# Attention, then two gated layers, on one core: q and k split together on GpSimd, with copies from SBUF to SBUF by DMA

## The reference

```python
scores = scale * np.matmul(q, k.transpose(0, 1, 3, 2))
scores = np.where(block_i >= block_j, scores, -1000000000.0)
scores = scores - np.max(scores, axis=-1, keepdims=True)
attn = np.exp(scores)
attn = attn / (np.sum(attn, axis=-1, keepdims=True) + 1e-09)
out = np.matmul(attn, v)

h = x @ w_in                                # layer 1
x = (h * np.clip(h + 3.0, 0.0, 6.0) / 6.0) @ w_out
h = x @ w2_in                               # layer 2
x = (h * np.tanh(np.log1p(np.exp(h)))) @ w2_out
```

## Time and profile before

| | us |
|---|---|
| median of 3 runs | 982.85 (982.0 to 983.21) |
| the profiled execution, its own time | 982.5 |
| its span, first to last instruction | 980.7 |
| TensorE busy (matmuls) | 949.2, 97% |
| VectorE busy | 761.2, 78% |
| ScalarE busy | 651.0, 66% |
| GpSimd busy | 446.6, 46% |

### The profile page before, as it was taken

One profiled execution on the slowest core, in us unless ns is written; L12 is line 12 of the kernel. 1 busy time (PEld: TensorE's weight loads), 2 busy tenths in 40 slices (PEclk: granted clock), 3 DMA queues, 4 the chain that ended last, 5 costly groups with the idle time before them and its releaser, 6 DMA issues.

```text
span 980.7 us, 17734 instructions
## 1 busy us (share of the span) xinstructions
PE 949.2 (97%) x6004; PEld 844.8 (86%) x6004; DVE 761.2 (78%) x1443; ACT 651.0 (66%) x1429; POOL 446.6 (46%) x409
## 2 busy tenths in 40 slices
PE   6988999999999999999999999999999999999998
PEld 5877888899888889988888988988988898998896
DVE  6999899967777576779897876777877777777654
ACT  6998899946544454554546457777777777776663
POOL 7887899876847586967776670000000000000000
PEclk9999999999999999999999999999999999999999
DMA  7878777765788977697777455455555654565255
GB/s 175 227 202 240 193 183 201 198 181 169 234 288 295 326 235 262 213 320 252 277 272 252 172 192 200 178 195 223 194 203 196 219 200 172 176 243 193 87 193 194
DMA packets 81913, 211.48 MB, mean 216 GB/s; under 512 B 12320, under 2 KB 19104, under 8 KB 81824
## 3 DMA queue, kind: packets, MB, share of 16 engines
q1 hardware_dynamic: 81744, 210.06, 65.7%
q10 hardware_dynamic: 80, 0.29, 0.1%
HBM read 170.39 MB, written 39.92 MB: 214 GB/s over the span
## 4 chain that ended last, share of the span: by engine, by line
PE 73%; DVE 5%; ACT 1%; issue 1%; DMA 1%; POOL 0%; SPq 0%; ACTq 0%; DVEq 0%
PE psum L957 36%; PE psum L840 11%; PE psum L842 11%; PE psum L841 11%; PE psum L790 1%; DVE ebuf L1511 1%; DVE glo L1517 1%; PE psum L769 1%; DMA ext_d<-ext_made 1%; DVE ext_made L1417 1%; PE psum L749 1%; DVE wraw L1402 0%; PE psum L750 0%; DVE wraw L1400 0%; DVE wraw L1398 0%
## 5 line engine op out<-in xcount | busy, mean ns | idle before, releaser
L957 PE MATMUL psum<-ghi,osplit 128*128 128x512 f32 (+1 forms) x640 | 215.9, 371 | 0.3 <-POOL osplit L1764 0.3
L840 PE MATMUL psum<-xhi,whi 128*128 128x256 f32 (+1 forms) x640 | 187.4, 293 | 2.1 <-ACT snap L1158 2.0
L842 PE MATMUL psum<-xhi,wlo 128*128 128x256 f32 (+1 forms) x640 | 186.8, 292 | 0.0
L841 PE MATMUL psum<-xlo,whi 128*128 128x256 f32 (+1 forms) x640 | 186.6, 292 | 0.0
L957 PE MATMUL psum<-osplit,ghi 128*128 128x512 f32 x576 | 180.9, 395 | 1.1 <-DVE glo L1517 0.8
L1517 DVE SCALAR_TENSOR_TENSOR glo<-ebuf,ghi 128x512 fp32r<-128x512 f32 x144 | 126.9, 881 | 25.0 <-ACT ghi L1206 16.9
L840 PEld LDWEIGHTS psum<-xhi,whi 128*128 128x128 f32 x640 | 120.8, 189 | 15.2 <-ACT snap L1158 3.6
L1764 POOL TENSOR_TENSOR osplit<-oraw,osplit 128x512 fp32r<-128x512 f32 x80 | 115.9, 1451 | 38.6 <-ACT osplit L1125 34.4
L1206 ACT ACTIVATE ghi<-ebuf 128x512 fp32r<-128x512 f32 x144 | 90.2, 627 | 64.3 <-DVE ebuf L1511 36.1
L957 PEld LDWEIGHTS psum<-ghi,osplit 128*128 128x128 f32 x640 | 117.9, 189 | 16.3 <-issue 0.5
L841 PEld LDWEIGHTS psum<-xlo,whi 128*128 128x128 f32 x640 | 120.8, 189 | 10.7
(11 more groups left out here) (108 smaller groups left out, 2175.5 us busy)
## 6 DMA issues: line engine op xcount, KB each, us to landing
ext<-ext_d SPq DMA_DIRECT2D x56, 768.0 KB, 4.4
osplit<-o_d SPq DMA_DIRECT2D x80, 512.0 KB, 5.4
oraw<-in_w_out SPq DMA_DIRECT2D x80, 256.0 KB, 5.8
qkin<-in_qk SPq DMA_DIRECT2D x63, 288.0 KB, 4.4
wraw<-in_w_in SPq DMA_DIRECT2D x32, 512.0 KB, 5.4
ext_d<-ext_made SPq DMA_DIRECT2D x32, 384.0 KB, 5.6
attn_t<-ostage SPq DMA_DIRECT2D x64, 144.0 KB, 3.2
o_d<-staged SPq DMA_DIRECT2D x32, 256.0 KB, 5.4
```

The lines of the kernel that those rows point to most:

```text
L840: pe.matmul(dst, hi, xh, start=(start and cc == 0), stop=False, skip_group_check=True)
L841: pe.matmul(dst, hi, xl, start=False, stop=False, skip_group_check=True)
L842: last = pe.matmul(dst, lo, xh, start=False, stop=(stop and cc == 1), skip_group_check=True)
L957: last = pe.matmul(bank(Y_BANK + c, n), stat, mov, start=(first and m == 0), stop=(final and m == 2), skip_group_check=True)
```

## The change

q and k of a head are loaded once, q into partitions 0 to 63 and k into 64 to 127 (one DMA of 288 KB). GpSimd makes the hi of both in one copy and the lo of both in one subtraction. Then q's hi is taken by ScalarE into `qs` (64 partitions), and three DMAs from SBUF to SBUF bring the rest to where the stacked operands want it: q's lo from `klo` to the upper half of `qs`; k's hi from the upper half of `khi` to the lower; k's lo from the upper half of `klo` to the lower (after the first one has landed, since it overwrites q's lo). `qs`, `khi` and `klo` have three buffers, and GpSimd works one head further ahead. Heads 0 and 1 are still made directly, from doubled loads; their k is staged in `ostage`. v is padded on the host and comes in one DMA. The four weight jobs are GpSimd's, one step earlier and over three steps each. The last exponential is over 576 columns.

```diff
-EARLY_JOBS = {3: 0, 6: 1, 9: 2, 12: 3}
+DIRECT = 2
+EARLY_JOBS = {2: 0, 5: 1, 8: 2, 11: 3}
-EARLY_X_ADD, EARLY_X_SCALE, EARLY_X_MIX = (12, 14, 16, 18), (13, 15, 17, 19), 20
-EARLY_X_HI, EARLY_X_LO = (21, 22, 23), (22, 23, 24)
-EARLY_LOADS = {0: 0, 1: 1, 4: 2, 7: 3, 10: 4, 13: 5}
+EARLY_X_ADD, EARLY_X_SCALE, EARLY_X_MIX = (14, 15, 16, 17), (15, 16, 17, 18), 19
+EARLY_X_HI, EARLY_X_LO = (20, 21, 22), (21, 22, 23)
+EARLY_LOADS = {0: 0, 2: 1, 5: 2, 8: 3, 11: 4, 14: 5}
...
 # SyncE
+            def load_qk(n):
+                if n - QK in range(DIRECT):
+                    sp.wait_ge(direct_q_lo[n - QK], 1)
+                elif n >= QK:
+                    sp.wait_ge(qk_lo, n - QK - DIRECT + 1)
+                    sp.wait_ge(q_hi, n - QK + 1)
+                sp.dma_start(qkin[n % QK][:, :], qk[n, :, :]).then_inc(qk_loaded[n % QK], 16)
+            def move_q_lo(n):
+                sp.wait_ge(qk_lo, n - DIRECT + 1)
+                s = n % QK
+                sp.dma_start(qs[s][DH:P, 0:SEQ].bitcast(F32), klo[s][0:DH, :].bitcast(F32)
+                             ).then_inc(q_lo_moved[s], 16)
+            def move_k_hi(n):
+                sp.wait_ge(qk_lo, n - DIRECT + 1)
+                s = n % QK
+                sp.dma_start(khi[s][0:DH, :].bitcast(F32), khi[s][DH:P, :].bitcast(F32)
+                             ).then_inc(k_hi_moved[s], 16)
+            def move_k_lo(n):
+                s = n % QK
+                sp.wait_ge(q_lo_moved[s], moves(n))
+                sp.dma_start(klo[s][0:DH, :].bitcast(F32), klo[s][DH:P, :].bitcast(F32)
+                             ).then_inc(k_lo_moved[s], 16)
             def load_v(n):
...
+                sp.dma_start(vin[n % 2][:, :, :], v_in[n, :, :, :]).then_inc(v_loaded[n % 2], 16)
...
-            load_qk(0, range(1))
-            load_qk(1)
+            sp.dma_start(ostage[0][:, :], qk_first[0, 1, :, :]).then_inc(k_loaded[0], 16)
+            load_qk(2)
+            sp.dma_start(qkin[1][:, :], qk_first[1, 0, :, :]).then_inc(qk_loaded[1], 16)
+            sp.dma_start(ostage[1][:, :], qk_first[1, 1, :, :]).then_inc(k_loaded[1], 16)
             load_v(0)
-            load_qk(2)
             load_v(1)
             for n in range(FIRST, NHEAD):
                 if QK <= n + 6 < NHEAD:
                     load_qk(n + 6)
                 if 2 <= n + 3 < NHEAD:
                     load_v(n + 3)
...                                   # x loads of steps 27 and 29 stand here
+                if DIRECT <= n + 3 < NHEAD:
+                    move_k_lo(n + 3)
                 if in_use(n) and n != LAST:
                     store_o(n)
+                if DIRECT <= n + 4 < NHEAD:
+                    move_q_lo(n + 4)
+                    move_k_hi(n + 4)
...                                   # inverse sums, weight loads, x loads of steps 9 and 10
 # TensorE, before scores(n, 0) of n >= 2
-                        pe.wait_ge(q_lo, n)
-                    pe.wait_ge(k_lo, n + 1)
+                    pe.wait_ge(q_hi, n + 1)
+                    pe.wait_ge(q_lo_moved[n % QK], moves(n))
+                    pe.wait_ge(k_hi_moved[n % QK], moves(n))
+                    pe.wait_ge(k_lo_moved[n % QK], moves(n))
...
 # ScalarE
+                rows = P if n < DIRECT else DH
+                nc.scalar.activation(qs[n % QK][0:rows, 0:SEQ], qkin[n % QK][0:rows, :], ACT.Copy).then_inc(q_hi, 1)
...
-                dst = prob[s][:, POFF[i]:POFF[i] + PW[i]]
+                dst = prob[s][:, POFF[i]:POFF[i] + min(PW[i], SEQ)]
...
-                if in_use(n + 3) and n >= -1:
-                    split_q_hi(n + 3)
+                if n == -1:
+                    split_q_hi(2)
+                if in_use(n + 4) and n >= -1:
+                    split_q_hi(n + 4)
-                if n in EARLY_JOBS:
-                    split_res_hi(EARLY_JOBS[n])
...
 # GpSimd
+            def split_qk_hi(n):
+                pool.wait_ge(qk_loaded[n % QK], 16 * (n // QK + 1))
+                if n >= QK:
+                    pool.wait_ge(direct_q_lo[1], 1)
+                    pool.wait_ge(scores_ready, ST * (n - QK + 1))
+                nc.gpsimd.tensor_copy(khi[n % QK][:, :], qkin[n % QK][:, :]).then_inc(qk_hi, 1)
+            def split_qk_lo(n):
+                pool.wait_ge(qk_hi, n - DIRECT + 1)
+                nc.gpsimd.tensor_tensor(klo[n % QK][:, :], qkin[n % QK][:, :], khi[n % QK][:, :].bitcast(F32),
+                                        ALU.subtract).then_inc(qk_lo, 1)
...
             def attention_step(n):
+                if DIRECT <= n + 4 <= QK:
+                    split_qk_hi(n + 4)
+                    split_qk_lo(n + 4)
+                if n + 4 == DIRECT:
+                    split_second_k_lo()
+                    split_second_q_lo()
                 if in_use(n + 1):
                     split_v_hi(n + 1)
...
                     split_v_lo(n + 1)
+                if n in EARLY_JOBS:
+                    mix_early(EARLY_JOBS[n])
+                    split_early_hi(EARLY_JOBS[n])
+                for half in range(2):
+                    if n - 1 - half in EARLY_JOBS:
+                        split_early_lo(EARLY_JOBS[n - 1 - half], half)
...                                   # the steps on x
-                if in_use(n + 3) and n + 3 > 0:
-                    split_k_lo(n + 3)
-                    split_q_lo(n + 3)
+                if QK < n + 4 < NHEAD:
+                    split_qk_hi(n + 4)
+                    split_qk_lo(n + 4)
```

More of the change, by code:

```diff
@@ L218, in ahead_at, with own, moves, build @@
     return [t for t in range(FT) if AHEAD_STEP[t] == s]
-MIXED = [sum(3 if e else 1 for _, _, _, e in JOBS[:m]) for m in range(len(JOBS) + 1)]
-def build(nc, qk, v_main, v_tail, w_in, w_out, out):
+MIXED = [sum(3 if e else 1 for _, _, _, e in JOBS[NEARLY:m]) for m in range(len(JOBS) + 1)]
+def own(m):
+    return m - NEARLY
+def moves(n):
+    return 16 * ((n - DIRECT) // QK + 1)
+def build(nc, qk, qk_first, v_in, w_in, w_out, out):
     ctx = ExitStack()
@@ L570, in load_ahead @@
                 elif t in (8, 9):
[L571 removed]
+                    sp.wait_ge(w_lo, own(2 * PAIRS - 1 + t % 2))
                 if t >= 2 and t not in (8, 9):
@@ L627, in load_x @@
                         return
-                    sp.wait_ge(w_lo, len(JOBS))
+                    sp.wait_ge(w_lo, own(len(JOBS)))
                     for i in range(2):
@@ L1413, in split_ext_lo @@
                 layer, p = JOBS[m][0:2]
-                dve.wait_ge(w_hi, m + 1)
+                dve.wait_ge(w_hi, own(m + 1))
                 if layer * PAIRS + p > 0:
```

170 lines of the change are left out of this document (86 added, 84 removed).

## The result

The changed kernel took 994.0 us (median of 4 runs, 989.68 to 994.48), the kernel before 983.03 in the same rounds: a ratio of 1.0101, 95% interval 1.007 to 1.0132. It is slower by about 10 us (by the ratio; 11 by the medians); the forecast was 980.2, and the range ended at 989. The profiled execution is the shortest of the four, 989.68 us with a span of 987.9, against 982.5 and 980.7. The 7.2 us between the spans lie as follows: the first long call of `attend` starts at 19.34 instead of 18.45 us (+0.9), the thirty heads behind it take 185.02 instead of 178.96 (+6.1), and from there to the end nothing moved (+0.2).

What follows compares the result with a forecast made beforehand. TensorE was taken as the bound, at 5.40 us a head. 15.4 us removed against 11.05 of new and uncovered losses gave -4.3, the start +1.6, so -2.7 from 982.85: 980.2 us, range 973.5 to 989.

Steps and rivals of the forecast that it cites:

- The bound and what the change removes: Run of heads: TensorE sets the pace at 5.40 us a head; the change removes 15.4 of 17.0 us lost.
- The start: Start of attention: `scores(2, 0)` at 18.0 instead of 17.22 us, +0.8 and half of a 1.7 us clock loss, +1.6.
- The issue times of the chain: SyncE's queue, 0.63 us an issue: first store at S + 6.25, q_lo at 7.5, k_hi at 8.15, k_lo at 10.05.
- k_lo's landing, 2.3 us: Moves: 2.3 us from issue to landing, ends 2.0 and 3.0; k_lo lands at S + 12.35, needed at 13.5.
- Weight loads, 0.4 in all: Six steps with one weight load of 512 KB ahead in the queue: 0 to 0.3 us each, 0.4 in all.
- The first rival: Moves too slow: two in series, needed 6.0 us after the first issue; 987 at 3.0 us each, 998 at 3.4; chance 0.22.
- x chunks: Steps 9 and 10, six issues each: k_lo 2.4 and 2.65 us late, 5.05 together, plus 1.7 for the clock.
- The inverse sums: Steps 7, 15 and 23: SyncE's five extra issues delay k_lo, 0.6 us each, 1.8 in all.
- the third reciprocal: VectorE in the run of heads: a loss covered before shows up once other losses are removed, 0.7 us.
- Step 27: Step 27: three issues before k_lo(30) cost 0.5 us.
- The largest term, 5.9 us for the jobs: Four weight jobs around heads 3-4, 6-7, 9-10, 12: moving them off VectorE and ScalarE removes 5.9 us.
- SyncE's 7 issues: SyncE issues 7 DMAs a head instead of 6, taking 4.4 of 5.4 us.

Runs made afterwards that it cites:

- e12: e6 with the four weight jobs back on VectorE and ScalarE in steps 3, 6, 9, 12: 982.79 us, 0.9989 of the kernel before.
- e3: The changed kernel with the four weight jobs back on VectorE and ScalarE: 990.88 us, 1.008 of the kernel before.
- e6: The changed kernel with k_lo moved twice into its own tile, no wait for q_lo, all moves ahead of stores and loads: 981.98 us, 0.9985 of before.
- e9: e6 with the four x chunks loaded one a step in steps 9 to 12: 980.61 us, 0.9966 of the kernel before.
- e2: The changed kernel with the six early weight loads put behind the next step's k_lo move: 990.68 us, 1.0067 of the kernel before.
- e1: The changed kernel with q_lo and k_hi moves ahead of the stores, k_lo right behind the stores, before the loads: 986.76 us, 1.0028 of before.
- e18: The changed kernel's tiles and chain, x chunks as e8, order q_lo, k_hi, q/k and v loads, k_lo, weight load, chunk, stores: 982.65 us, 0.9982 of before.
- e8: The changed kernel with the four x chunks loaded one a step in steps 9 to 12: 990.44 us, 1.0064 of the kernel before.
- e5: The changed kernel with k_lo issued ahead of its step's loads, q_lo and k_hi still behind the stores: 995.94 us, 1.011 of the kernel before.
- e16: e6 without its new order, every move issued where the changed kernel has it: 1009.8 us, 1.0249 of the kernel before.
- e10: e9 with the x chunks in steps 9, 10, 12 and 13: 986.31 us, 1.0029 of the kernel before.
- e14: e6 with each weight load in two halves in two steps: 990.4 us, 1.0055 of the kernel before.
- e17: e6 with x chunks in steps 9 to 12 and SyncE's step list ordered moves, loads, stores: 990.06 us, 1.006 of the kernel before.
- e7: The changed kernel with its three moves issued from GpSimd in a queue of their own: 1019.3 us, 1.0374 of the kernel before.

## Why the prediction was wrong, step by step

- **The bound and what the change removes: right.** GpSimd is no longer late, VectorE and ScalarE have the jobs off them, a steady head takes 5.40 us. That the jobs cost some 5.7 us is seen again in e12; in e3 TensorE's waits for `ptlo` come to 3.1 us (20 to 205 us).
- **The start: right in the delay, too dear by the clock.** `scores(2, 0)` was put at 18.0 and came at 18.17 (17.22 before); the half of a lowered clock that was added (0.85) didn't come: +1.6 was said, +0.9 came. Head 0 was 1.4 us early (`scores(0, 0)` at 7.18 us): VectorE's two subtractions took 0.76 and 1.10 us, and not 1.84. Executions differ here more than the term: in e6, e9 and e12 TensorE never waits between 14.7 us and the first long `attend`, and gets there at 19.9 to 20.5: in e9 two scores matmuls of 288 columns still follow each other at 0.24 us at 17.5 us, in the changed kernel at 0.13 at 16.4, though the granted clock is given as 1.00 for both. What slows them is open.
- **The issue times of the chain: right.** q_lo was put at S + 7.5 and goes at 7.4 to 8.0 in quiet heads, k_lo at 10.05 and goes at 9.8 to 10.8 (in 28 steps read one by one; S is TensorE's start of the step).
- **k_lo's landing, 2.3 us: the step that failed.** It was taken from a store alone in the queue, with "The queue isn't fuller in time" as the reason. In the mean that reason holds (DMA share 0.69 in the quiet head, 0.66 in the one of the earlier trace rows). But the list puts the q/k and v loads straight ahead of k_lo in every head, and it lands in 2.9 us at the median behind these two and in 4.2 behind a further load, 3.4 in all. The lone value was right for the two moves that have only the stores right ahead (2.5). 1.1 us of spare became about 0.3 in the quiet heads, which lose nothing, and less than nothing in the others: k_lo is needed at 13.5 and lands between 12.8 and 15.8. The row to take was the store under load, 3.0 us, or a v load behind a q/k load.
- **Weight loads, 0.4 in all: 7.6 measured.** This is where most of that failure is paid. Their 512 KB ahead of k_lo were named, and priced as if 1.1 us of spare stood against them: k_lo lands in 4.1 to 5.2 us behind them. e2, which only moves them behind the next k_lo, gives about 3.3 us back.
- **The first rival: near in time, partly by luck.** "Moves too slow" had 987 at 3.0 us each and 998 at 3.4 each, with a chance of 0.22; measured were 994. But its condition was that both landings together take more than 6.0 us, in series. They are 2.5 + 3.4 = 5.9, and q_lo's landing isn't in the chain: what counts is k_lo's own landing behind its issue, and in single heads.
- **x chunks: the stall about right, split wrongly, and the clock counted on top.** 5.05 was said for the two stalls and 1.7 for the clock, 6.75 together. Measured were 5.2 with the clock in it: waits of 3.23 and 0.43 us, where 2.4 and 2.65 were said, and the rest behind them at the low clock. The other low stretch followed the wait of 2.05 us at head 2, behind a weight load, which the prediction didn't have.
- **Other terms of the run of heads.** The inverse sums were put at 1.8 and cost 1.9 (heads 9, 17 and 25), the third reciprocal at 0.7 and cost 0.7 (head 24): right. Step 27 was put at 0.5 and cost 1.5 (head 28). The w_out loads of steps 19 to 21 had no term; heads 21 to 23 lose 2.6 us, 2.2 of it in waits for k_lo behind such a load, where 0.9 was said for x copies there. Head 6 loses 1.0 us, where the issue of one v load ahead of k_lo took 2.25 us. All in all the heads lose 6.1 us more than before, and 4.3 less were forecast; weight loads make 7.2 of these 10.4, the low stretch of head 3 1.4.
- **The largest term, 5.9 us for the jobs: gone when it was added.** The sum treated it as independent of the waits for moves. e12 against e6 shows that it isn't: time that TensorE loses to a job is time in which a late move lands. Of 5.7 us 1.0 is left.
- **SyncE's 7 issues: the right count, the wrong question.** 4.4 of 5.4 us are used, and still SyncE's order was the cost: the moves stand behind a wait for this step's own `attend`. The prediction had this in its S + 6.25 for the first store, and took it as given.
- **The two other prices of a move.** The 253 GB/s of the earlier trace rows are no rate of one transfer over 64 partitions: a load to each half of them was in flight in that window. The lone store of the earlier trace rows moved at 196 GB/s (before, 200.9 to 201.5 us), which does agree with the 218 GB/s beside it. The section of the Trainium skill that the 2.0 us fixed are taken from (DMA: Bandwidth & Descriptors, "Anatomy of one DMA") is on DMAs that GpSimd issues, and these are SyncE's. The estimate of 2.7 us is still only 0.2 from the 2.5 measured without loads ahead; neither it nor the lone store has in it what loads ahead add.

Shown: the order of SyncE's list is the larger part of the cost. With q_lo and k_hi ahead of the stores and k_lo ahead of the loads 7 us come back (e1); with everything ahead of the stores and k_lo still behind the loads 8.1 (e18 against e8, of which the new place of the weight loads may be up to 3.3), and the kernel is then 0.2% faster than before, near what was forecast; with k_lo ahead of the loads but all moves behind the stores, nothing (e5). With one move more in every head the place makes 26 us (e6 against e16). The wait for q_lo by itself is not the cost (e16, e18), though SyncE stands in it for 36.7 us in e1, 42.2 in e5 and still 25.6 in e18. That k_lo lands late behind loads is shown; what this alone costs is not, since every run that shortened it moved something else too. Only argued: how the 23.0 us divide among queue, order and clock head by head. Open: why e10 and e14 are 6 and 7 us slower than e9 and e6, though e14's profiled execution, the fastest of its ten, has a span only 3.9 us longer.

## What to carry to other kernels

Where a copy between two engines' tiles becomes a DMA, price it by a row that has the same neighbours ahead of it, not by the emptiest row of its size, and draw the loop that leads back to its own issue. In a list that one engine works off in order, whatever waits for this step's results goes last, and what the next steps need goes ahead of it, unless it then waits itself for something that the loads behind it must feed (e17). A saving on a secondary engine isn't added to the sum before it is asked what else was using the time it cost.

## What was not expected of the hardware

- A move of 144 KB within SBUF lands in 2.4 to 2.5 us with two stores of the same size right ahead of it and no load on its way (q_lo, seven of eight heads; 3.6 in the eighth), in 2.9 (median) behind 448 KB of q/k and v loads, and in 4.2 (median) with a further load ahead. In a second queue, issued 0.3 us behind a q/k load in the first, it took 3.6 to 5.6 (e7). That the queues share what serves them is the likely reading, and wasn't tested by itself.
- One more move (an issue of 0.6 us and 144 KB) in each step of a closed loop came with 14.6 us over 29 heads (e16 against the change).
- SyncE's issues, 0.45 to 0.6 us each, are at times stretched to 1.4 to 2.5 us (in the changed kernel a v load at 51.21 us took 2.25, k_lo at 157.2 us 2.52); what stretches them wasn't tried.
- The length of one wait of TensorE doesn't tell whether the clock falls. In the changed kernel the granted clock fell to the 1.2 GHz level behind waits of 2.05 and 3.23 us; before, behind the one of 2.78 us. In e18 a wait of 1.68 us left it at full speed (88 to 92 us: granted clock 1.00). But in e5 it fell behind a wait of 1.72 us (61.4 to 64.8 us: 0.51) and not behind one of 2.17 us (120.8 to 124.2 us: 1.00).
